# Decays of the queries by broadcast loads, two log-weight banks and a later finish in the first attention half

## The reference

```python
for t in range(S):
    kt, vt, qt = (k[:, :, t], v[:, :, t], q[:, :, t])
    m_new = np.maximum(f_gate[:, :, t] + m, i_gate[:, :, t])
    f_stab = np.exp(f_gate[:, :, t] + m - m_new)
    i_stab = np.exp(i_gate[:, :, t] - m_new)
    m = m_new
    C = f_stab[:, :, None, None] * C + i_stab[:, :, None, None] * np.einsum('bhd,bhe->bhde', vt, kt)
    n = f_stab[:, :, None] * n + i_stab[:, :, None] * kt
    h_tilde = np.einsum('bhde,bhe->bhd', C, qt)
    nq = np.einsum('bhd,bhd->bh', n, qt)[:, :, None]
    denom = np.maximum(np.abs(nq), 1.0)
    o = 1.0 / (1.0 + np.exp(-o_gate[:, :, t]))
    y[:, :, t] = o * h_tilde / denom
...
h = np.maximum(xt @ w_tok1, 0.0) @ w_tok2
u = x + h.transpose(0, 2, 1)
h2 = np.maximum(u @ w_ch1, 0.0) @ w_ch2
```

## Time and profile before

| | |
|---|---|
| median of 3 runs | 381.36 us (380.81 to 381.92) |
| the profiled execution's own time | 380.41 us |
| its span in the profile | 378.6 us |
| PE busy | 369.9 us, 98% |
| DVE, ACT, POOL busy | 189.5, 149.9, 110.9 us |
| granted TensorE clock | 1.00, so 2.4 GHz throughout |
| DMA busy, from 44 to 62 us | 101.8% of the 16 engines (packets overlap a little) |

### The profile page before, as it was taken

How to read it: one execution, slowest core, us unless ns; L and a number is a source line. 1 busy time by engine, 2 the same in 40 slices (tenths; PEclk the granted TensorE clock), 3 DMA queues, 4 the chain that set the end, 5 groups by cost and what they waited for, 6 DMA issues and landing times.

```text
span 378.6 us, 6173 instructions
## 1 busy us (share of the span) xinstructions
PE 369.9 (98%) x2411; PEld 357.5 (94%) x2411; DVE 189.5 (50%) x391; ACT 149.9 (40%) x307; POOL 110.9 (29%) x107
## 2 busy tenths in 40 slices
PE   8998999999999999999999999999999999999997
PEld 3788998999999999999999999999999999999996
DVE  7888665555253252055931585448924484341421
ACT  5678798568342241012550144514433201330310
POOL 6258788548132000000193000723570000000000
PEclk9999999999999999999999999999999999999999
DMA  7978899532130000022022000523040001001000
GB/s 153 249 190 218 262 304 254 144 105 93 42 108 17 19 0 0 19 84 88 3 87 71 0 2 6 221 71 137 3 138 19 2 1 36 17 2 36 16 19 35
DMA packets 17024, 30.95 MB, mean 82 GB/s; under 512 B 2452, under 2 KB 7700, under 8 KB 16996
## 3 DMA queue, kind: packets, MB, share of 16 engines
q1 hardware_dynamic: 16084, 29.64, 27.1%
q0 software_dynamic: 192, 0.66, 0.6%
q10 hardware_dynamic: 720, 0.27, 0.3%
HBM read 26.60 MB, written 3.96 MB: 81 GB/s over the span
## 4 chain that ended last, share of the span: by engine, by line
PE 84%; DVE 3%; ACT 3%; POOL 1%; issue 1%; ACTq 0%; DVEq 0%; POOLq 0%
PE ps L641 30%; PE ps L618 23%; PE ps L621 4%; PE ps L620 4%; PE ps L500 4%; PE ps L727 4%; PE ps L476 3%; PE ps L576 3%; PE ps L554 2%; PE ps L745 2%; PE ps L594 2%; PE ps L485 2%; POOL m_lo L1421 1%; PE ps L510 1%; PE ps L462 1%
## 5 line engine op out<-in xcount | busy, mean ns | idle before, releaser
L927 ACT ACTIVATE h_hi<-ps 128x384 fp32r<-128x384 f32 x88 | 43.3, 492 | 115.9 <-PE ps L621 115.9
L1172 DVE SCALAR_TENSOR_TENSOR h_lo<-ps,h_hi 128x384 fp32r<-128x384 f32 x88 | 48.5, 555 | 55.4 <-ACT h_hi L927 54.9
L1178 DVE TENSOR_TENSOR xt<-ps,xt 128x320 f32<-128x320 f32 x24 | 11.8, 491 | 69.1 <-PE ps L641 69.1
L641 PE MATMUL ps<-ch_hi,h_hi 128*128 128x320 f32 x144 | 45.5, 316 | 0.0
L641 PE MATMUL ps<-ch_hi,h_lo 128*128 128x320 f32 x144 | 44.5, 309 | 0.0
L641 PE MATMUL ps<-ch_lo,h_hi 128*128 128x320 f32 x144 | 44.5, 309 | 0.0
L641 PE MATMUL ps<-m_hi,h_hi 128*128 128x320 f32 x120 | 37.4, 312 | 0.6 <-POOL m_lo L1421 0.6
L641 PE MATMUL ps<-m_hi,h_lo 128*128 128x320 f32 x120 | 37.1, 309 | 0.0
L641 PE MATMUL ps<-m_lo,h_hi 128*128 128x320 f32 x120 | 37.1, 309 | 0.0
L618 PE MATMUL ps<-uT_hi,ch_hi 128*128 128x384 f32 x96 | 33.0, 344 | 0.5 <-DVE h_lo L1172 0.5
L1421 POOL TENSOR_TENSOR m_lo<-m_raw,m_hi 128x640 fp32r<-128x640 f32 x11 | 18.1, 1669 | 50.9 <-ACT m_hi L794 50.9
(11 more groups left out here) (164 smaller groups left out, 882.7 us busy)
## 6 DMA issues: line engine op xcount, KB each, us to landing
kq<-in_kq SPq DMA_DIRECT2D x24, 192.0 KB, 4.9
ch_raw<-in_ch SPq DMA_DIRECT2D x11, 384.0 KB, 5.3
vk<-in_vk SPq DMA_DIRECT2D x12, 328.0 KB, 4.6
m_raw<-in_m SPq DMA_DIRECT2D x11, 320.0 KB, 4.2
og<-in_o SPq DMA_DIRECT2D x12, 160.0 KB, 4.7
x_scratch<-xt SPq DMA_DIRECT2D x12, 160.0 KB, 1.8
out<-xt SPq DMA_DIRECT2D x12, 160.0 KB, 1.8
tok_raw<-in_tok SPq DMA_DIRECT2D x4, 384.0 KB, 7.0
```

The source lines that it names most:

```text
L641: mm = pe.matmul(bank, h[hx][:, f, i * P:(i + 1) * P], w[wx][:, f], start=(f == 0 and hx == 0 and wx == 0), stop=(f == FCH[k] - 1 and hx = ...
L927: act.activation(h[0][:, f], h_bank(k, f), ACT.Relu).then_inc(hhi_done, 1)
L1172: dve.scalar_tensor_tensor(out=h[1][:, f], in0=h_bank(k, f), scalar=0.0, in1=f32(h[0][:, f]), op0=ALU.max, op1=ALU.subtract).then_inc(hlo_ ...
L1178: dve.tensor_tensor(xt[:, tile], o_bank(n), xt[:, tile], ALU.add).then_inc(o_done, 1)
```

## The change

Six things change in batch 0's attention. `decays` on PE, `decay(cc)` on ACT and the selection matrix with its load go. ACT instead writes exponentials into g_ea in three parts of two chunks each (`decay(n)`), SP stores each part and loads eAb for chunks 1 to 5 as it did for batch 1. The loads of eAb leave `load_scaled` and become `load_decays(cc)`, which stands behind `load_kv(cc)`; `load_qk(cc + 1)` now stands ahead of `load_kv(cc)`. This order holds for all chunks, those of batch 1 too. The log-weights of groups 0 to 11 take banks 2 and 7 in turn, and the copy of the mask for the next group stands ahead of W on ACT. On DVE `finish` of the last chunk moves behind the scores of the odd group. Four of the nine gate steps of part 2 move from DVE to POOL.

```diff
-GATE_AT = {1: (0,), 2: (1, 2), 3: (3, 4, 5), 4: (6,), 5: (7, 8)}
+GATE_AT = {1: (0,), 3: (3,), 4: (6,), 5: (7, 8)}
+POOL_GATE_AT = {1: (1, 2), 3: (4, 5)}
...
+STORE_AT = {2: 1, 4: 2, 6: 3}
...
+    def d_bank(n):
+        return BANK[(2, 7)[n % 2] if n < NG // 2 else 2]
+
+    def d_free(n):
+        return n - 1 if n <= NG // 2 else n
...
+            def load_decays(cc):
+                b, c, t = cc // NC, cc % NC, cc % 2
+                if c == 0:
+                    return
+                sp.wait_ge(st_ea[PART_OF[c] if b == 0 else len(GATE_PARTS)], 16)
+                if cc <= 2:
+                    sp.wait_ge(zero_ready, 5)
+                if cc >= 3:
+                    sp.wait_ge(inter_done, inter_count(cc - 2))
+                    sp.wait_ge(c_scaled, scaled_count(cc - 2))
+                for r in range(2):
+                    half = slice(64 * r, 64 * r + D)
+                    decay = ea_d[b, c, BP * r:BP * r + BP].rearrange("p t -> (p t)").partition_broadcast(D)
                     sp.dma_start(eAb[half, t].rearrange("p a t -> p (a t)"), decay).then_inc(ld_qs[t], 16)
...
+            store_decays(0)
+            load_decays(1)
             load_qk(2)
             for cc in range(2, NCC):
-                if cc == NC:
-                    store_decays()
                 load_scaled(cc)
                 load_o(cc)
-                load_kv(cc)
                 if cc + 1 < NCC:
                     load_qk(cc + 1)
+                if cc in STORE_AT:
+                    store_decays(STORE_AT[cc])
+                load_kv(cc)
+                load_decays(cc)
...
-                if g == 0 and c < NC - 1:
-                    decays(c + 1)
...
+            def decay(n):
+
+                rows_, cols = ((slice(0, H), slice(*GATE_PARTS[n])) if n < len(GATE_PARTS)
+                               else (slice(32, 32 + H), slice(0, S)))
+                if n < len(GATE_PARTS):
+                    act.wait_ge(gate_step, gates_at(n, 4))
+                act.activation(g_ea[rows_, cols], g_A[rows_, cols], ACT.Exp).then_inc(ea_ready, 1)
...
+                if n + 1 < NG // 2:
+                    masked(n + 1)
                 act.wait_ge(logw_done, n + 1)
...
-                rest(n)
+                if n % 2 == 0:
+                    rest(n, (0,))
+                else:
+                    rest(n - 1, (1,))
```

More of the change, by code:

```diff
@@ L228, in build @@
     ld_rows = sem("ld_rows")
-    st_ea, st_out = sem("st_ea"), sem("st_out")
+    st_ea = [sem(f"st_ea{n}") for n in range(len(GATE_PARTS) + 1)]
+    st_out = sem("st_out")
     st_x2 = [sem("st_x2_0"), sem("st_x2_1")]
@@ L304, in qs_count @@
     def qs_count(cc):
-        return sum((32, 64)[e // NC] for e in range(cc + 1) if e % NC and e % 2 == cc % 2)
+        return sum(64 for e in range(cc + 1) if e % NC and e % 2 == cc % 2)
     def piece(n):
@@ L527, in step @@
                     products(n + 1)
-            def decays(cc):
-                t = cc % 2
-                if cc == 1:
-                    pe.wait_ge(sel_ready, 1)
-                pe.wait_ge(spread_r, r_count(cc))
-                if cc >= 2:
-                    pe.wait_ge(ea_done, cc - 1)
-                for g in range(2):
-                    for r in range(2):
-                        mm = pe.matmul(EA_BANK[:, 2 * g * CH:2 * (g + 1) * CH], sel[:, g], R[:, t, r:4:2],
-                                       start=(r == 0), stop=(r == 1))
-                mm.then_inc(decay_done, 1)
             def mix_tokens(b, c, parts=range(2)):
@@ L784, in pattern @@
                                ACT.Copy).then_inc(rl_ready, 1)
-            def select():
-                act.wait_ge(ld_sel, 16)
-                act.activation(sel[:, :, :], sel_raw[:, :, :], ACT.Copy).then_inc(sel_ready, 1)
             def split_hi(n):
@@ L867, in attend @@
                     gates_hi(1)
+                    decay(1)
                 if n == 2:
@@ L871, in attend @@
                     gates_hi(2)
+                    decay(2)
                 if n == 6:
@@ L878, in attend @@
                 if n == 9:
-                    act.activation(g_ea[32:32 + H, :], g_A[32:32 + H, :], ACT.Exp).then_inc(ea_ready, 1)
+                    decay(3)
                 if g == 0 and cc >= 1:
@@ L935, in _ @@
             spread(0)
+            decay(0)
             pattern(1)
@@ L1437, in attend @@
                     scale_q(cc)
+                for step in POOL_GATE_AT.get(n, ()):
+                    gate_rows(step)
                 if g == 1 and 1 <= c < NC - 1:
@@ L1520 @@
             roles[first + n, 4 + rho[n] // 4] = 1.0
-    sel = np.zeros((P, 2, P), np.float32)
-    for first in (0, 32):
-        for n in range(H):
-            sel[first + n, n % BP // 2, 64 * (n // BP):64 * (n // BP) + 64] = 1.0
     later = np.tril(np.ones((P, P), bool), -1)
@@ L1533 @@
         "seq": seq, "chan": chan, "ident": np.eye(P, dtype=np.float32),
-        "turned": np.array([[NC * (P - 1 - p) + j for j in (4, 5)] for p in range(P)], np.int32), "roles": roles, "sel": sel.reshape(P, 2 * P),
+        "turned": np.array([[NC * (P - 1 - p) + j for j in (4, 5)] for p in range(P)], np.int32), "roles": roles,
         "mask": np.where(later, np.float32(NEG), np.float32(0)),
```

84 lines of the change are left out of this document (35 added, 49 removed).

## The result

The changed kernel took 392.41 us (median of 4 runs, 391.12 to 393.19) against 381.09 us (380.64 to 381.92) before on the same chip: 1.029 times as long, 95% interval 1.026 to 1.033. The forecast was 383.9 us, at most 385.6. The sign was right, the size was not: +11.3 us instead of +2.5. Two executions of later runs, one of p1 (455.14 us, mean clock 0.755) and one of after_filled (397.05 us), were in a slow state and are left out of all comparisons. The profiled execution took 391.12 us, its span is 389.3 us.

What follows compares the result with a forecast made beforehand. PE, busy for 98% of the span, was taken as the bound. Middle 0 plus chunk 7's 2.7, a little less if PE comes early, gave +2.5: 382.9 against the profiled 380.41, 383.9 as a median; range 381.8 to 385.6 us.

Steps and rivals of the forecast that it cites:

- The sign: Whole kernel: slower than before, chance 0.73, against 0.14 for the same and 0.13 for faster.
- Start, products(4) at 22.8: Batch 0's start: kq(2) queues behind the store's landing at 18.0, so PE starts products(4) 2.3 us late.
- the row that the prediction kept: Loading kq(2): profile row by which the second half lands up to 3.6 us after issue on a quiet queue.
- I take 0 as PE's lateness at group 12: Middle of batch 0's half: late start and saved decays cancel along a chain over DVE and ACT; between -1.8 and +1.
- Gate steps on POOL: Each moved step, estimated at 0.6 us, fits into POOL's DMA waits; cost nothing, at most 0.5 without that cover.
- `finish` moved: Middle chain: finish(1), 1.7 us, behind group 5's scores; ACT's mask at 37.9 instead of 37.2, PE 0.7 late before decays(5).
- eAb(7) behind kq(8): Chunk 7: eAb(7) lands at 61.8 instead of 58.2, delaying x_lo(5) and batch 0's last mixer matmuls; +2.7 us left.
- The other loads of eAb and vk in batch 1: Also behind the next kq, but their readers come 4 us or more after the landings; cost nothing.
- Added bytes: Chunk 7's upper bound: eAb(5) adds 160 KB to the full queue, 0.8 us at 200 GB/s, making 3.5.
- Rival 4: Slower by more: og(2), vk(2) and the chain late up to group 12, or x_lo(4) delayed; 385.2 to 387, chance 0.13.
- eAb on 8 engines: Chunk 7: by a skill rule eAb's 40 rows use 8 engines, a pair takes some 0.7 us longer; sum +3.4.

Runs made afterwards that it cites:

- p1: Kernel before with decays by loads in e5's SP order, two log-weight banks and the earlier mask copy; DVE's and POOL's orders as before: 386.81 us, 1.015.
- after_filled: Changed kernel plus unread matmuls, twelve ahead of in_chunk(12) and eight ahead of batch 0's last mixer part: 391.0 us, 1.027.
- e2: Changed kernel with the stores of parts 1 and 2 of g_ea issued earlier: 387.73 us, 1.021.
- e3: Changed kernel with gate step 6 of part 2 (the cast of g_i into g_bh) on ACT instead of DVE: 390.43 us, 1.024.
- b2: Kernel before with only the four gate steps of part 2 moved to POOL: 382.89 us, 1.003.
- u1: Changed kernel with the four gate steps back on DVE: 391.75 us, 1.032.
- b1: Kernel before with only finish moved behind the scores of the odd group: 384.91 us, 1.008.
- e1: Changed kernel with SP's order for chunks 6 to 11 put back to that of before: 386.96 us, 1.016.
- e6: Changed kernel with the loads of eAb for chunks 1 to 5 bringing 8 rows instead of 40, state part incomplete: 387.53 us, 1.015.
- lone program: Also called alone: separate program without the kernel's work, timing DVE operations with POOL idle or busy, and PE matmuls behind growing pauses; no kernel time.
- e5: e4 with kq(2), qs(2) and og(2) issued ahead of the first loads of eAb: 387.72 us, 1.018.
- p2_filled: p2 with eleven unread matmuls put into PE's long wait: 384.24 us, 1.007.
- b1_rows_on_act: b1 with R of chunks 2 to 5 made by four activations on ACT instead of one DVE operation: 384.46 us, 1.009.
- e4: Changed kernel with the edits of e1, e2 and e3 together: 384.49 us, 1.010.
- u2: Changed kernel with finish back ahead of the scores of the odd group: 392.27 us, 1.031.
- p2: p1 with one log-weight bank and the mask copy behind W, so the decays by loads alone: 386.60 us, 1.017.

## Why the prediction was wrong, step by step

- *Start, products(4) at 22.8.* Mechanism right, size too large: 21.24. The store landed by 16.3, not 18.0, because the token loads took 7.8 to 8.2 us instead of the 8.7 to 10.2 of the earlier trace rows. +0.8 instead of +2.3. The two loads of kq(2) landed 3.1 and 3.8 us after their issue, so the row that the prediction kept was right. The section of the Trainium skill that it names beside the row gives its 2 us for DMAs that GpSimd issues; these were issued by SP.
- *"I take 0 as PE's lateness at group 12"*, between -1.8 and +1. This step failed. Group 12's log-weights started at 48.56 before and at 51.24 after: +2.7. Two things were missing. The chain took every DVE duration as it is where DVE loses no time to POOL; the cast of 0.4 us took 3.0, R 2.1 instead of 0.7. And of SP I had followed only the first of three waits for a store: they sum to 15.0 us, the last one put og(5) at 43.15, ACT waited 3.9 us for it until 48.66, and R of chunk 6 came late behind that. e2 and e3 removed the one and the other, and each gave part of it back later.
- *Gate steps on POOL: "they cost nothing".* Wrong when alone: b2 splits into runs at 381.5 and at 384.5. In the changed kernel no cost of theirs shows (u1).
- *`finish` moved.* Its lateness for ACT was costed, its effect on what DVE does next to POOL was not: b1, +3.3 us.
- *eAb(7) behind kq(8).* Right in every link: issued behind products(13), POOL idle 4.95 us, x_lo, then PE idle 1.92 where about 3 was forecast; the 0.67 us ahead of in_chunk(14) gone. From the first issue to POOL's start it took 4.8 us instead of 5.4, but all of it stood later than in the forecast (issue at 63.29, not 56.4, by 6.9 us), since PE was late.
- *"The other loads of eAb and vk in batch 1 ... I cost them at nothing."* This failed too, one chunk earlier: vk(6), behind kq(7) and the store of part 3, was issued at 50.04 and took 9.3 us: 3.07 us of wait at 59.42, the longest of all. e1 took 2.0 us of it away, and the wait of 1.9 us for x_lo of chunk 5, and in its profiled execution the half clock too.
- *Added bytes: eAb(5)'s 160 KB, 0.8 us, in the upper bound only.* All ten loads came to 800 KB, and e6, with 640 of them gone, is 4.9 us faster.
- *The clock* was no term at all: every wait was priced at its length. Here two waits cost 3.4 us more in the profile, about 2 in the runs.
- *Rival 4* named late og(2), vk(2) and the chain staying late up to group 12; the chain was late there, by 2.7 us, though not from the late start, which was only 0.8. The price of 385.2 to 387 was too low, for it left out vk(6) and the clock.
- *eAb on 8 engines, "+3.4".* By the rule that the prediction took from the Trainium skill, 40 rows would run on 10 engines, the largest number up to 16 that divides 40, and not on 8. The added 0.7 us would then be some 0.45 (an estimate, from the prediction's own 0.9 us for 192 KB), and the sum +3.15. The profile doesn't show on which engines a load ran.

The page "SBUF — State Buffer" of the Trainium skill, section "Who interferes with whom", has DVE and GpSimd share one pair of ports. By it a DVE operation with two inputs in SBUF, or a copy, cast or tensor_scalar in a mode that uses both ports, contends with a GpSimd operation that reads SBUF, and the one that holds the ports blocks the other fully. The lone program's rows agree: each of the three kinds is about 1 us longer, and the product with a PSUM input isn't. It would have made this change suspect at once. The kernel's rows go beyond it: R in b1 lasted 3.83 us, over four POOL operations, AB in e5 5.21 us, where the lone program's DVE got its turn after one. Why it loses several turns is open; I have no run that separates it.

The page "TensorE: Matmul & The Clock Gate" of the Trainium skill, section "HAM oscillation — how this bites in real kernels", says that waits for DMA between groups of matmuls can bring the clock down again. The windows at 0.50 behind the waits, p2_filled and the lone program agree. The length of a wait alone doesn't say when: the clock fell behind 1.92 us in the changed kernel and not behind 3.37 us in e3.

Shown by experiments: SP's order (e1, e2), the size of the added loads (e6), the DVE stretch as cause of single waits (e3, b1_rows_on_act, alone), idle time as cause of the half clock (p2_filled, alone). Not settled: how e6's and e2's gains overlap, why the clock falls behind one wait and not behind another, where the last 3 us of e4 come from, and the several lost turns of DVE. That eAb's loads ran on fewer engines, the Trainium skill's rule in the prediction, was not separated: in the same stretch the pair took 4.8 us to POOL's start and kq 2.9 to 3.6.

## What to carry to other kernels

Moving a step on VectorE moves what it does beside GpSimd's rows: for every operation of VectorE that is moved, look whether it reads only on-chip memory (two inputs, a cast, a tensor_scalar) and what GpSimd runs then. A store that is read back stands as a wait in the issuing queue each time it occurs, so follow every one of them to the load behind it, not just the first. A wait of TensorE can cost more than its length, by the half clock behind it, or less, where a later wait would have swallowed it. That is how I read u1 and u2, which gave nothing back, while undoing SP's order did.

## What the runs showed of the hardware that I had not expected

- A 40x256 cast on VectorE took 0.31 us with GpSimd idle and 1.27 us within its row; in the kernel up to 3.0 us. A product with a PSUM operand wasn't touched.
- GpSimd pays as well: its 104x512 product took 1.27 us alone and 1.74 us with such a VectorE product beside it.
- TensorE's clock fell to half after waits of 1.9 us (the changed kernel) to 3.4 us (e5) in the kernels, for 3.4, 6.8, 10.2 or 13.6 us, and after 2.99 us but not after 2.33 us in the lone program. In p2 and e5 it fell about 1 us before the wait ended. In the kernels it didn't fall after each such wait: it stayed at 1.00 after a kq wait of 1.84 us and an S wait of 2.07 us in the changed kernel, and after waits of 3.37 and 2.75 us in e3.
- Matmuls whose result nobody reads kept it at 2.4 GHz in all eleven executions of p2_filled. Eight of them ahead of a wait that still lasted 2.72 us (after_filled) did not.
